# A fused conv, rational MLP and relu-squared MLP on one core: one block of layer 2's second product a unit instead of two, row tiles from unit 11 on, and y taken out at another place

## What is computed

```python
# 1: causal convolution of 7 taps per head, softmax of the weights over the taps
w = softmax(weight, axis=-1)                 # 8 heads x 7 taps
x = einsum('hk,bskhg->bshg', w, windows_of_7(x))

# 2: layer 1, rational activation
h = x @ w_in1                                # 192 -> 2048
P = a[0] + a[1]*h + a[2]*h**2 + a[3]*h**3
Q = 1.0 + abs(b[0])*abs(h) + abs(b[1])*h**2
x = (P / (Q + 1e-6)) @ w_out1                # 2048 -> 192

# 3: layer 2, squared relu
h = x @ w_in2                                # 192 -> 2048
g = s * maximum(h, 0)**2 + b
y = g @ w_out2                               # 2048 -> 192
```

## Time and profile before

| what | value |
|---|---|
| median of 3 runs | 1235.62 us (1235.34 to 1236.71) |
| profiled execution | 1235.03 us |
| its span in the trace | 1233.2 us |
| TensorE busy | 1216.2 us, 99% |
| VectorE busy | 1081.7 us, 88% |
| ScalarE busy | 1081.0 us, 88% |
| GpSimd busy | 382.9 us, 31% |
| chain that ended last, TensorE's share | 91% |
| TensorE clock granted | 0.999 of full |

### The profile page before, as it was taken

One profiled execution on the slowest core, in us unless ns is written; L12 is line 12 of the kernel. 1 busy time (PEld: TensorE's weight loads), 2 busy tenths in 40 slices (PEclk: granted clock), 3 DMA queues, 4 the chain that ended last, 5 costly groups with the idle time before them and its releaser, 6 DMA issues.

```text
span 1233.2 us, 25178 instructions
## 1 busy us (share of the span) xinstructions
PE 1216.2 (99%) x10722; PEld 1083.8 (88%) x10722; DVE 1081.7 (88%) x957; ACT 1081.0 (88%) x1128; POOL 382.9 (31%) x196
## 2 busy tenths in 40 slices
PE   8998999999999999999999999999999999999999
PEld 5666889898988999998999998899898998999898
DVE  7998799998999999998999989999899998888810
ACT  7998898989889898899988999898998899888843
POOL 3444333224223242232422333223323333232200
PEclk9999999999999999999999999999999999999999
DMA  7200000001000100001000000001000000000000
GB/s 229 62 2 24 2 1 14 2 14 27 14 1 2 40 1 15 1 1 40 1 14 2 14 28 1 14 2 27 13 15 1 1 15 1 15 1 14 2 14 14
DMA packets 14832, 21.63 MB, mean 18 GB/s; under 512 B 1792, under 2 KB 9984, under 8 KB 14592
## 3 DMA queue, kind: packets, MB, share of 16 engines
q1 hardware_dynamic: 14576, 20.01, 5.5%
q10 hardware_dynamic: 144, 0.01, 0.0%
HBM read 13.72 MB, written 6.29 MB: 16 GB/s over the span
## 4 chain that ended last, share of the span: by engine, by line
PE 91%; DVE 5%; issue 1%; ACT 1%; DMA 1%; SPq 0%; POOL 0%; DVEq 0%; ACTq 0%; POOLq 0%
PE o L663 23%; PE h L641 20%; PE h L635 19%; PE o L647 13%; PE o_tail L653 8%; PE o L503 3%; DVE work L1120 1%; DVE work L1088 1%; DVE work L1127 1%; DVE work L1094 1%; DVE work L1091 1%; DMA work<-in_moe_w_out_dram 1%; PE h L495 1%; PE h L496 1%; PE h L485 1%
## 5 line engine op out<-in xcount | busy, mean ns | idle before, releaser
L443 POOL TENSOR_TENSOR gl<-work,gh 128x1024 fp32r<-128x1024 f32 x126 | 304.0, 2413 | 487.6 <-ACT gh L872 485.8
L663 PE MATMUL o<-v,work 64*128 64x192 f32 x3584 | 332.1, 322 | 0.0
L663 PEld LDWEIGHTS o<-v,work 64*128 64x128 f32 x3584 | 310.4, 186 | 12.0
L862 ACT ACTIVATE work<-h,coef 128x1024 f32<-128x1024 f32 x128 | 154.1, 1204 | 87.9 <-PE h L635 83.1
L1088 DVE SCALAR_TENSOR_TENSOR work<-work,coef,h 128x1024 f32<-128x1024 f32 x128 | 163.7, 1279 | 74.7 <-ACT work L863 73.3
L1131 DVE SCALAR_TENSOR_TENSOR work<-work,coef 128x1024 f32<-128x1024 f32 x128 | 164.4, 1285 | 4.5
L1094 DVE SCALAR_TENSOR_TENSOR work<-work,coef,h 128x1024 f32<-128x1024 f32 x128 | 163.9, 1281 | 4.5
L1120 DVE SCALAR_TENSOR_TENSOR work<-work,coef 128x1024 f32<-128x1024 f32 x128 | 166.4, 1300 | 0.8 <-ACT work L867 0.8
L1127 DVE SCALAR_TENSOR_TENSOR work<-work 128x1024 f32<-128x1024 f32 x128 | 156.8, 1225 | 4.4
L899 ACT ACTIVATE work<-h 128x1024 f32<-128x1024 f32 x128 | 129.8, 1014 | 32.6 <-PE h L496 32.3
L954 ACT ACTIVATE work<-work,coef 128x1024 f32<-128x1024 f32 x128 | 146.9, 1148 | 11.3 <-POOL gl L443 9.3
(11 more groups left out here) (142 smaller groups left out, 2711.2 us busy)
## 6 DMA issues: line engine op xcount, KB each, us to landing
out_dram<-y_out SPq DMA_DIRECT2D x32, 192.0 KB, 2.1
xt<-in_x_main_dram SPq DMA_DIRECT2D x7, 518.0 KB, 4.6
xt_tail<-in_x_tail_dram SPq DMA_DIRECT2D x8, 259.0 KB, 4.6
work<-in_moe_w_out_dram SPq DMA_DIRECT2D x2, 768.0 KB, 9.1
v<-in_moe_w_out_dram SPq DMA_DIRECT2D x1, 1536.0 KB, 7.4
raw_w_tail_late<-in_moe_w_in_dram SPq DMA_DIRECT2D x4, 256.0 KB, 6.6
work<-in_moe_w_in_dram SPq DMA_DIRECT2D x2, 512.0 KB, 6.2
xt<-in_x_main_dram SPq DMA_DIRECT2D x2, 259.0 KB, 6.4
```

Of the source, the lines that this page charges most:

```text
L443: nc.gpsimd.tensor_tensor(gl[:, j % 2, :], r_buf[j % 2], gh[:, j % 2, :].bitcast(F32), ALU.subtract).then_inc(gl_ready, 1)
L663: last = pe.matmul(o2[:, bank, c, 0:D], g2[buf_out][rows, col:col + P], v2[rows, f, :], start=(f == 0 and c == 0 and turn == 0), stop=(f = ...
```

## The change

Three things, and one that follows from them.

- unit_by_rows is used from unit 11 on (ROWS_FROM = EARLY + 1) instead of from unit 16 on.
- In a step, layer 2's second product is one block right behind layer 1's first product: the last rows of unit m - 3 and then the first rows of unit m - 2. Which half of the array writes which bank changes from one unit to the next (n modulo 2), so that within a block nothing turns. In the step where a new tile begins (k_out = 0, j = 5) only the last rows stand there, and the first rows of the new tile come behind the lower half of layer 1's second product, with the wait for y_ready_out.
- Y_STEP becomes 5, and y is taken out ahead of z in the step instead of behind t3.
- In unit_by_rows the third partial product of layer 2's first product (at = 2) stands behind layer 1's second product. Unit 128 does the last rows of unit 114 ahead of the full-array product of unit 115.

All counts are Python integers already, so the lines that drop isinstance change nothing. The diff, cut to its core:

```diff
+    ROWS_FROM = EARLY + 1
-    Y_STEP = (SKEW + OUT2_LAG + UNITS - 1) % UNITS
+    Y_STEP = (SKEW + OUT2_LAG) % UNITS
...
-        def by_rows(t):
-            return not isinstance(t, int) or 2 <= t < TILES
+        def by_rows(n):
+            return ROWS_FROM <= n < NU
...
+            def rows_of_second_2(k, buf, lower_bank, first):
+                for half in range(2):
+                    f = 2 * k + half
+                    for c in range(2):
+                        for bank in range(2):
+                            rows = LOWER if bank == lower_bank else UPPER
+                            col = half * TOK + (2 * bank + c) * P
+                            last = pe.matmul(o2[:, bank, c, 0:D], g2[buf][rows, col:col + P], v2[rows, f, :],
+                                             start=(f == 0 and c == 0 and first), stop=(f == FT - 1 and not first),
+                                             skip_group_check=True)
+                return last
+
+            def first_rows_of_second_2(n, m):
+                q = m - OUT2_LAG
+                pe.wait_ge(g2_ready, q + 1)
+                rows_of_second_2(q % UNITS, q % 2, n % 2, True).then_inc(o2_turned, 1)
+
+            def last_rows_of_second_2(n, m):
+                q = m - OUT2_LAG - 1
+                pe.wait_ge(o2_turned, q + 1)
+                rows_of_second_2(q % UNITS, q % 2, n % 2, False).then_inc(out2_done, 1)
...
-                if k_out == 0:
-                    pe.wait_ge(y_ready_out, counted((t + (j - SKEW - OUT2_LAG) // UNITS) * 2))
-                pe.wait_ge(out2_done, counted(m - OUT2_LAG))
-                pe.wait_ge(g2_ready, counted(m - OUT2_LAG + 1))
-                second_2(0).then_inc(o2_turned, 1)
-                pe.wait_ge(u_ready, counted(m))
-                for at in range(3):
-                    if k2 == 0 and at == 0:
-                        pe.wait_ge(x2_hi_ready, counted(t2 + 1))
-                    if k2 == 0 and at == 2:
-                        pe.wait_ge(o2_turned, counted(since + 1))
-                        second_2(1).then_inc(out2_done, 1)
-                        pe.wait_ge(x2_lo_ready, counted(t2 + 1))
+                if unit(m - OUT2_LAG - 1):
+                    last_rows_of_second_2(n, m)
+                if unit(m - OUT2_LAG) and k_out != 0:
+                    first_rows_of_second_2(n, m)
...
+                pe.wait_ge(u_ready, m)
+                if k2 == 0:
+                    pe.wait_ge(x2_hi_ready, t2 + 1)
+                for at in range(2):
                     first_2(0, False, at)
                     first_2(1, True, at)
...
-                if k2 != 0:
-                    pe.wait_ge(o2_turned, counted(since + 1))
-                    second_2(1).then_inc(out2_done, 1)
+                if unit(m - OUT2_LAG) and k_out == 0:
+                    pe.wait_ge(y_ready_out, (m - OUT2_LAG) // UNITS * 2)
+                    pe.wait_ge(conv_copied, 3)
+                    pe.wait_ge(v2_loaded, 16)
+                    first_rows_of_second_2(n, m)
...
                 if k2 == 0:
-                    pe.wait_ge(x2_tail_hi_ready, counted(t2 + 1))
-                    pe.wait_ge(x2_tail_lo_ready, counted(t2 + 1))
+                    pe.wait_ge(x2_lo_ready, t2 + 1)
+                first_2(0, False, 2)
+                first_2(1, True, 2)
+                if k2 == 0:
+                    pe.wait_ge(x2_tail_hi_ready, t2 + 1)
+                    pe.wait_ge(x2_tail_lo_ready, t2 + 1)
...
+                        if n == NU:
+                            last_rows_of_second_2(n, m)
                         second_product_of_layer_2(t, j, m, k2)
...
+                    if j == Y_STEP and tile(t - 2):
+                        ...   (the y block, moved here from behind t3)
                     h_flat = h2_flat if in_h2(n) else h1_flat
                     if unit(n):
                         dve.wait_ge(t_ready, counted(n + 1))
```

More of the change, by code:

```diff
@@ L72, in pair_exists @@
     def pair_exists(i):
[L73 removed]
+        return i < TPB
     def tokens(i, batch):
@@ L316, in load_x @@
             def load_x(pair):
-                sp.wait_ge(conv_summed, 2 if isinstance(pair, int) and pair == 1 else 5)
+                sp.wait_ge(conv_summed, 2 if pair == 1 else 5)
                 sp.wait_ge(tail_step, counted(tail_steps(pair - 1)))
@@ L654, in tail_of_second_1 @@
                                      start=(k == 0 and upper and at == 0), stop=(k == UNITS - 1 and not upper and at == 3))
-                def second_2(turn):
-                    for half in range(2):
-                        f = 2 * k_out + half
-                        for c in range(2):
-                            for bank in range(2):
-                                rows = (LOWER, UPPER)[(bank + turn) % 2]
-                                col = half * TOK + (2 * bank + c) * P
-                                last = pe.matmul(o2[:, bank, c, 0:D], g2[buf_out][rows, col:col + P], v2[rows, f, :],
-                                                 start=(f == 0 and c == 0 and turn == 0), stop=(f == FT - 1 and turn == 1),
-                                                 skip_group_check=True)
-                    return last
                 if j == 0:
@@ L758, in phase @@
                     t2 = t + (j - SKEW) // UNITS
[L760 removed]
+                    if by_rows(n):
                         unit_by_rows(n, j, t, parity, m, k2, t2)
                         continue
[L764 to L765 removed]
+                    early = n < EARLY
+                    if unit(n) and not (n <= EARLY):
                         product_of_layer_1(n, j, t, parity)
@@ L874, in convolved @@
             def convolved(pair):
-                if isinstance(pair, int) and pair == 1:
+                if pair == 1:
                     act.wait_ge(conv_copied, 2)
```

90 lines of the change are left out of this document (45 added, 45 removed).

## The result

The changed kernel takes 1239.1 us (median of 14 runs, 1238.01 to 1240.81) against 1235.73 us for the kernel before (14 runs, 1233.82 to 1238.01) on the same chip: a ratio of 1.0028, 95% interval 1.002 to 1.0036. That is 3.4 us slower, where the forecast was 2.9 (1238.5 against 1235.62). The profiled execution of it took 1240.39 us, with a span of 1238.6.

A forecast was written before the change was run, and what follows sets the result against it. TensorE and a second loop through ScalarE and VectorE both bind, at 9.00 us a unit. The terms -0.4 + 3.5 - 1.7 + 1.3 + 0.3 give +3.0 us on 1235.03; forecast 1238.5 us, range 1232.8 to 1241.5.

The forecast's parts named there:

- the hole at j = 5: Where a new tile of y begins, TensorE waits 0.42 us for VectorE to take y out.
- Both loops bind: In a steady unit, TensorE's work and the loop through ScalarE and VectorE both take 9.00 us, to within 0.05 us.
- The term of -0.4 us: One block instead of two in each unit saves an entry and an exit: 0.4 us in all, ends 0 and 2.2.
- H: Start of the last matmul of the first product, from which the times in step j = 5 are counted.
- The tile's sum: Units j = 3 to 5 go from 27.71 to 27.96 us: +0.25 a tile, +3.5 us for 14 tiles.
- The slow end given there, +5.6: Slow end for the 14 tiles: the lag of one half stays and the hole is 0.5 us.
- Rival 1: Hole at j = 5 largely covered, by row halves running ahead or a shorter round trip: 1234 to 1236.5 us, chance 0.26.
- Rival 3: Wait for o1_turned uncovered if its 0.68 us of cover lack 0.1: +10 us, 1248 us, chance 0.06.
- The start: Row tiles from unit 11 on gain 1.7 us, ends 0.4 and 2.2, with unit 16 starting near 142.0.
- Rivals 2 and 4: 2: no hole, looser second loop, 1231.1 us, chance 0.17; 4: x2's chain sets units 12 to 16, 1240.2 us, chance 0.06.
- The end: Unit 128's added half block costs 1.3 us, and two more changes of the array's mode 0.3 us.
- The chances: Chances given for the measured time against the kernel before: slower 0.45, same 0.38, faster 0.17.

The follow-up runs named there:

- pair_left_out: y_hole_covered with one pair of matmuls of layer 2's first product left out in every unit by rows; 1230.38 us, ratio 0.9963.
- y_longer: Changed kernel with one more VectorE operation between the two y operations of a row tile; 1245.81 us, ratio 1.0088.
- y_hole_covered: Changed kernel with a new tile's first rows moved behind two and a half more pairs of layer 2's first product; 1232.74 us, ratio 0.9984.
- y_hole_one_pair: Changed kernel with a new tile's first rows behind one more pair of matmuls only, layer 2's third partial product; 1235.02 us, ratio 0.9997.
- the second group: Runs changed_again, y_hole_one_pair, pair_left_out and before_h1_turn_covered, beside the kernel before on the same chip, whose median there was 1235.7 us.
- the third: Third group of runs: y_longer, changed_filled and best_filled, beside the kernel before on the same chip, whose median there was 1235.02 us.
- changed_filled: Changed kernel with six useless matmuls ahead of the wait for x2 in unit 11 and again at the end of unit 12; 1237.92 us, ratio 1.0021.
- changed_again: The changed kernel run once more without an edit, against the kernel before; 1238.45 us, ratio 1.0027.
- best_filled: before_h1_turn_covered with the same six useless matmuls in units 11 and 12; 1228.85 us, ratio 0.9948.
- before_h1_turn_covered: Kernel before with row tiles from unit 11, third partial product later, and one second-product pair ahead of h1's turn at j = 3; 1229.24 us, ratio 0.9954.
- before_rows_from_11: Kernel before with only the row tiles from unit 11 on, two blocks a unit and y in step j = 4 as before; 1232.01 us, ratio 0.9978.

## Why the prediction was right, point by point

The time (1238.5 forecast, 1239.1 measured), its sign and its mechanism, the hole at j = 5, held. That the number came so close is in part luck: at a full clock in both kernels the change costs 4.1 to 4.5 us and not 2.9, as the last point shows.

- *Both loops bind.* Held: a pair less for TensorE leaves the steady units at 9.00 (pair_left_out), and a hole in it counts in full (y_longer). But two terms of the second loop were off and cancelled: 0.055 us and not 0.15 from the third step to a waiting TensorE, and 2.41 and not 2.33 for a first product behind a wait. The term of -0.4 us was 0. Its source, 0.02 us for an entry and an exit, isn't in the rows: 16 pairs of passes take 2.59 us in one block and 2.60 in two.
- *The hole at j = 5.* Held in its place and its chain: y begins at H + 1.79 (forecast 1.76), ends at H + 2.93 (2.90), and the next rows begin at H + 2.99 (3.05). The forecast took 0.15 us from VectorE's end to TensorE's start; here too it is 0.06. The gap is 0.31 and not 0.42. In exchange the block behind it takes 0.11 longer. The unit is at 9.51 to 9.56 in the mean of the traces, against 9.38.
- *The tile's sum.* +0.31 us instead of +0.25, so that 14 tiles cost 4.3 and not 3.5. The term that was mis-sized is what unit j = 5 takes without its hole. The prediction took the 0.11 us by which one half lags as gone, and so went from 9.11 down to 8.96. The lag is still there at the start of unit 68 (the pair at 618.78 lasts 0.50 us), and with the hole covered (y_hole_covered) unit j = 5 takes 9.06. Part of this comes back at j = 3, 9.48 instead of 9.60, where only 0.02 were counted. The slow end given there, +5.6, is 14 x 0.44 = 6.2 by its own terms.
- *Rival 1, row halves running past the wait.* Fell. The Trainium skill, TensorE: Matmul & The Clock Gate, Part 2, first step, has matmuls stay in program order. At this wait the trace agrees: the next pair that was free to run, behind the rows of the new tile, starts at 634.42, after them. Between the halves it doesn't, as the prediction saw in the earlier trace rows: one half can start ahead of earlier matmuls of the other where no wait stands between. y_hole_one_pair shows the same from the other side: only a pair put ahead of the wait in the program shortens the hole.
- *Rival 3, the wait for o1_turned.* Fell: no main matmul of the turned half in unit 69 starts late, and with the hole covered the whole unit takes 9.06 us. Three starts of cover, 0.68 us, are enough. The 0.55 us that the rival named as the limit was tried by no run; where nothing covers a turn, in unit 67 of the kernel before, it takes 0.49 us from start to start (608.96 to 609.45).
- *The start.* At equal clock -1.9 us, forecast -1.7, and unit 16 follows unit 11 by 45.70 us (forecast 45.9). In the order of the kernel before the whole is -2.9 in the medians, since executions with a low clock became rare, which the forecast didn't have.
- *Rivals 2 and 4.* No steady unit came down to 8.95, and the start did give its part: both fell.
- *The end.* +1.7, forecast 1.6. The Trainium skill, TensorEngine Tiling (Array Packing), Key Properties, has a change of the tiling mode drain the engine. The rows show a pause that fits: 0.32 us from the last row matmul at 1167.50 to the first full one, and 0.33 back at 1170.34, where the pitch is 0.23. Whether the array was empty they don't show. The prediction took the change in the earlier trace rows for the only one in the trace before; there is a second, from rows to full array behind 1163.90, with 0.32 and 0.34 us, and the price is the same. No run tried the end alone.
- *The chances.* Two thirds of the forecast's 0.45 and rivals 3 and 4 make 0.42 for slower, not 0.45.
- *The sum, and the luck in it.* At a full clock in both kernels the measured terms give 4.3 - 1.9 + 1.7 = 4.1. The runs agree, as far as there are such runs of the kernel before: in the second group 1238.06 us (5 runs of the changed kernel at 0.998 or more) against 1234.01 (one run), in the third 1237.92 (changed_filled) against 1233.47 (one run), 4.1 and 4.5. The medians differ by only 3.4 and 2.7. That fits the clocks: 54 of the 61 runs of the kernel before in the three groups are below 0.998, and only 9 of the 22 of the changed kernel. The forecast had no term for this. At equal clock its terms, +3.0, are 1.1 to 1.5 us too low.

## What to carry to other kernels

When a resource changes hands between two engines once a tile, write down both sides from one common instruction: the round trip of the other engine, and the work that the first engine has beside it. Their difference is the hole, and each matmul put ahead of the wait takes its own length off it, until it is gone; here two and a half pairs turned a loss of 3.4 us into a gain of 2.2. A saving in an engine that is busy for 98% of the span can be worth nothing where a second loop has the same length, so close both loops in figures before you count a saving. And take a latency only from a place where the engine behind it really waited: a distance that the engine's own work sets says nothing of it. Where the work of one half of an array is used as cover, look what it does to the other half at the next turn.

## What the runs showed of the hardware that was not expected

- *Low-clock stretches that come and go.* The same program shows them in one execution and not in another. In the traces they are 3.4 or 6.8 us long, with TensorE at half its clock (0.50 in the windows), and apart from one at 22 to 40 us in every trace they lie at 100 to 109 and at 114 to 119 us, where TensorE stands for 1 to 2.4 us at a time, as in the earlier trace rows. One costs 1 to 1.5 us: 10.86 against 9.57 us in unit 11. They follow such gaps, but a gap alone doesn't decide: changed_again has one of 1.86 us ahead of unit 13 and keeps the full clock. With the fillers in two of the gaps 16 of 16 runs have a mean clock of 0.998 or more, as runs without a low stretch there have in the traces (11 of changed_filled, 5 of best_filled), against 13 of 22 of the changed kernel and 3 of 5 of before_h1_turn_covered. That points at the gaps. But before_rows_from_11 had 10 of 11 without any filler, so what decides in one execution stays open.
- *A block behind a wait runs slower.* 1.57 us for 16 fp32 passes behind a wait or a change of mode, 1.46 in a full queue. It stands at a gap of 0.10 us as well as at one of 0.86. The first product of layer 1 shows the like: 2.41 us in the steady units of pair_left_out, where TensorE waits, and 2.33 in unit 66 of the kernel before, where it doesn't.
- *A wait is followed within 0.06 us.* TensorE starts 0.055 us behind the end of VectorE's third step (pair_left_out) and 0.055 behind the end of y (the changed kernel), in the means.
- *The halves run apart.* Where nothing holds them together, the matmuls of one row half start ahead of earlier ones of the other: in unit 67 of the kernel before two main matmuls of the lower half stand in the program before the tail matmul of 614.46, and they start later.
- *Cover that splits the halves.* Filling a hole of 0.41 us gave 0.13 us a row tile, 0.07 at j = 3 (9.51 to 9.44) and 0.06 at j = 5. From the cover on the two row halves are 0.25 us apart at the next block; that this took the rest is likely and not shown.
